# Up products by Strassen's algorithm on pairs of token chunks, with eight retention units ahead of the first product

## The reference

```python
state = gamma * state + einsum('bhd,bhe->bhde', k[:, :, t], v[:, :, t])
y[:, :, t] = scale * einsum('bhd,bhde->bhe', q[:, :, t], state)
# x = y, laid out as 3072 x 512
h = x @ w_in;  g = h * cos(h);  x = g @ w_out            # layer 1
h = x @ w_in                                             # layer 2
g = where(h >= 1, h, where(h <= -1, 0, (h + 1) ** 2 / 4))
out = g @ w_out
```

## Time and profile before

| what | value |
|---|---|
| median of 3 runs | 1165.73 us (1165.51 to 1165.99) |
| profiled execution, span | 1163.8 us |
| instructions in the profile | 14906 |
| PE, DVE, ACT, POOL busy | 1151.9, 556.8, 380.4, 132.4 us |
| mean granted TensorE clock | 0.997 of 2.4 GHz |
| DMA moved | 74.57 MB, 64 GB/s |

### The profile page before, as it was taken

One profiled execution on the slowest core, in us unless ns is written; L12 is line 12 of the kernel. 1 busy time (PEld: TensorE's weight loads), 2 busy tenths in 40 slices (PEclk: granted clock), 3 DMA queues, 4 the chain that ended last, 5 costly groups with the idle time before them and its releaser, 6 DMA issues.

```text
span 1163.8 us, 14906 instructions
## 1 busy us (share of the span) xinstructions
PE 1151.9 (99%) x5892; PEld 943.1 (81%) x5892; DVE 556.8 (48%) x836; ACT 380.4 (33%) x606; POOL 132.4 (11%) x113
## 2 busy tenths in 40 slices
PE   7999999999999999999999999999999999999998
PEld 5888888888888888788788888888888888888887
DVE  5555555556556555555554433433433433433433
ACT  2444332333333333323555322222222222222222
POOL 4445011001001010100354000000000000000000
PEclk8999999999999999999999999999999999999999
DMA  6433212022113112220452301001101001000100
GB/s 230 160 111 128 73 54 74 19 102 63 37 35 112 44 48 91 73 73 1 145 172 64 145 1 73 37 1 73 37 1 73 36 0 72 36 0 0 37 1 37
DMA packets 35481, 74.57 MB, mean 64 GB/s; under 512 B 3936, under 2 KB 4064, under 8 KB 33888
## 3 DMA queue, kind: packets, MB, share of 16 engines
q1 hardware_dynamic: 35424, 73.75, 18.7%
HBM read 54.86 MB, written 18.87 MB: 63 GB/s over the span
## 4 chain that ended last, share of the span: by engine, by line
PE 97%; DMA 1%; DVE 1%; SPq 0%; ACT 0%; issue 0%; DVEq 0%
PE up L378 45%; PE acc L401 23%; PE acc L403 22%; PE att L339 2%; PE att L318 2%; PE att L335 2%; PE att L359 1%; DMA raw<-in_w1u 0%; DMA q_sb<-in_q_t 0%; DVE x_lo L532 0%; PE acc L318 0%; PE att L354 0%; DVE am L471 0%; DVE x_lo L481 0%; DVE q_sb L461 0%
## 5 line engine op out<-in xcount | busy, mean ns | idle before, releaser
L378 PE MATMUL up<-x_hi,wu_hi 128*128 128x512 f32 x768 | 299.6, 390 | 1.1 <-DVE g_raw L514 1.1
L378 PE MATMUL up<-x_lo,wu_hi 128*128 128x512 f32 x768 | 298.8, 389 | 0.0
L378 PE MATMUL up<-x_hi,wu_lo 128*128 128x512 f32 x768 | 298.8, 389 | 0.0
L523 DVE SCALAR_TENSOR_TENSOR g_lo<-g_raw,g_hi 128x512 fp32r<-128x512 f32 x192 | 137.3, 715 | 181.9 <-ACT g_hi L608 181.9
L608 ACT ACTIVATE g_hi<-g_raw 128x512 fp32r<-128x512 f32 x192 | 121.3, 632 | 192.7 <-PE acc L403 108.8
L378 PEld LDWEIGHTS up<-x_hi,wu_hi 128*128 128x128 f32 x768 | 144.1, 188 | 32.8 <-DVE g_raw L514 2.5
L378 PEld LDWEIGHTS up<-x_hi,wu_lo 128*128 128x128 f32 x768 | 144.1, 188 | 30.0
L378 PEld LDWEIGHTS up<-x_lo,wu_hi 128*128 128x128 f32 x768 | 144.2, 188 | 29.7
L401 PE MATMUL acc<-g_hi,wd_hi 128*128 128x512 f32 x384 | 156.1, 406 | 0.0
L401 PE MATMUL acc<-g_hi,wd_lo 128*128 128x512 f32 x384 | 150.1, 391 | 0.0
L401 PE MATMUL acc<-g_lo,wd_hi 128*128 128x512 f32 x384 | 149.9, 390 | 0.0
(11 more groups left out here) (57 smaller groups left out, 899.5 us busy)
## 6 DMA issues: line engine op xcount, KB each, us to landing
q_sb<-in_q_t SPq DMA_DIRECT2D x24, 256.0 KB, 4.0
k_sb<-in_k_t SPq DMA_DIRECT2D x24, 256.0 KB, 4.0
x_hi_scratch<-x_hi SPq DMA_DIRECT2D x24, 256.0 KB, 3.0
x_lo_scratch<-x_lo SPq DMA_DIRECT2D x24, 256.0 KB, 3.4
x_hi<-x_hi_scratch SPq DMA_DIRECT2D x6, 1024.0 KB, 4.8
x_lo<-x_lo_scratch SPq DMA_DIRECT2D x6, 1024.0 KB, 6.9
kn<-in_k_n SPq DMA_DIRECT2D x22, 256.0 KB, 2.9
v_sb<-in_v_n SPq DMA_DIRECT2D x20, 256.0 KB, 2.6
```

Source lines behind the costliest of these rows:

```text
L378: last = nc.tensor.matmul(up[j % 2][:, :], w[:, j, k, :], x[:, par, k, :], start=(k == 0 and x is x_hi and w is wu_hi), stop=(k == KT - 1 ...
L523: nc.vector.scalar_tensor_tensor(out=g_lo[:, s, :], in0=g, scalar=2.0 if layer == 1 else 1.0, in1=g_hi[:, s, :].bitcast(F32), op0=ALU.mult ...
```

## The change

The unit of work becomes a *round*: two chunks of tokens in one layer (three rounds in layer 1, then three in layer 2, `s` in the code). The tokens of the two chunks, the two halves of the contraction and the two halves of the hidden features make a 2x2 by 2x2 block product, which is done by Strassen's algorithm in Winograd's form: 7 block products for 8. A *quad* (`q`, 8 in a round) is the four hidden tiles of feature tiles q and q+8 for both chunks. Its 7 products have 2 contraction tiles of three matmuls, 6 matmuls each. Some results are summed by PE in PSUM (p2 on p1, p7 and p4 on p6, p3 on p5), others by DVE. The hidden tiles other than the first are now in SBUF.

- POOL forms three sums of weight blocks for each contraction tile (`t_sums`, four operations of 128x128) and the low part of all seven (`t_low`, 128x896). ACT writes the high part (`t_high`). The up weights are no longer kept: they are loaded and split again for each quad of each round. The down weights are still kept (`wd_high`, `wd_low`, 128x1024 at a time, in round 0 one beside each quad).
- POOL forms sums of x blocks (8 operations of 128x512 a round), ACT and DVE split 14 tiles a round (`split_high`, `split_low`).
- ACT copies p1 out of PSUM and does the `turns`, which DVE did before. DVE gets `sum_u2`, `sum_u3`, `sum_h22`, `sum_h21`, `sum_h12`.
- Down products of the first chunk run beside the quads (two in a quad, from the second quad on). The rest, the whole second chunk's among them, follow the quads as a *tail* of 18 down products; `late` holds the second chunk's g until then.
- Retention: eight units (two chunks) run ahead of round 0's first product, from their own buffers; in rounds 0 and 1, eight more run in the tail. The last four units don't update the state. Layer 1's output goes to HBM as one float32 tensor, and is split again when read back.

The diff is long; its core, with new functions in the form they have after the change:

```diff
-        def walk(eng, body):            # one chunk after the other, 16 tiles each
+PRODUCTS = ["p1", "p6", "p2", "p7", "p5", "p4", "p3"]
+TAIL = [(1, QUADS - 1), (2, LATE[0]), (2, LATE[1]), (1, FT - 1)] + [(2, f) for f in LATE[2:]]
+BETWEEN = [1, 1, 1, 1, 1, 1, 2]
 # PE
+            def product(s, q, name):
+                if q == 0:
+                    pe.wait_ge(xlo_done, NS * s + max(m for m in range(NS) if SPLITS[m][0] == name) + 1)
+                if name == "p2":
+                    pe.wait_ge(p1_copied, n + 1)
+                if name == "p7":
+                    pe.wait_ge(u2_done, n + 1)
+                if name == "p4":
+                    pe.wait_ge(u3_done, n + 1)
+                if name == "p3":
+                    pe.wait_ge(h22_done, n + 1)
...
+            for u in range(AHEAD):
+                outputs(u)
+                outer(u)
+                if u + 2 < AHEAD:
+                    scores(u + 2)
...
+                for q in range(QUADS):
+                    product(s, q, "p1")
+                    product(s, q, "p6")
+                    if q:
+                        down(s, 1, q - 1)
+                    product(s, q, "p2")
+                    product(s, q, "p7")
+                    product(s, q, "p5")
+                    if q:
+                        down(s, 1, q - 1 + QUADS)
+                    product(s, q, "p4")
+                    product(s, q, "p3")
+                tail = list(TAIL)
+                if s < PAIRS - 1:
+                    for _ in range(5):
+                        down(s, *tail.pop(0))
+                    scores(u)
+                    down(s, *tail.pop(0))
+                    for i in range(AHEAD):
+                        outputs(u + i)
+                        outer(u + i)
+                        if i + 1 < AHEAD:
+                            scores(u + i + 1)
+                            for _ in range(BETWEEN[i]):
+                                down(s, *tail.pop(0))
 # DVE
+            def finish(s, q):
+                angle(s, q, 2)
+                if q == QUADS - 1:
+                    gate_low(s, *TAIL[1])
+                angle(s, q, 3)
+            def quad(s, q):
+                if q:
+                    finish(s, q - 1)
+                sum_u2(s, q)
+                if q:
+                    gate(s, q - 1, 2)
+                    gate(s, q - 1, 3)
+                    gate_low(s, 1, q - 1 + QUADS)
+                angle(s, q, 0)
+                sum_u3(s, q)
+                gate(s, q, 0)
+                sum_h22(s, q)
+                gate_low(s, 1, q)
+                angle(s, q, 1)
+                gate(s, q, 1)
+                sum_h21(s, q)
+                sum_h12(s, q)
 # ACT
+            def quad(s, q):
+                if q:
+                    finish_turns(s, q - 1)          # turns 2, turns 3
+                copy_p1(s, q)                       # q == 0 waits for all 14 splits
+                if q == 0 and s:
+                    rows_second(s - 1)
+                if q:
+                    curve(s, q - 1, 2)              # Sin, Square
+                    curve(s, q - 1, 3)
+                    gate_high(s, 1, q - 1 + QUADS)
+                if more:
+                    t_high(2 * (QUADS * s + q + 1))
+                turns(s, q, 0)
+                curve(s, q, 0)
+                if more:
+                    t_high(2 * (QUADS * s + q + 1) + 1)
+                gate_high(s, 1, q)
+                turns(s, q, 1)
+                if s == 0:
+                    wd_high(0, q)
+                curve(s, q, 1)
 # POOL, for the next quad
+                        t_sums(i)
+                        t_sums(i + 1)
+                        t_low(i)
+                        t_low(i + 1)
+                    if s == 0:
+                        wd_low(0, q)
```

More of the change, by code:

```diff
@@ L405, in down_product @@
                         last.then_inc(rows_ready, 1)
-                if (layer, place) != (2, "last") or j < FT - 1:
+                if not (s == SPANS - 1 and half == 2 and closes):
                     last.then_inc(down_done, 1)
-            def retention(blk, layer, place, j):
-                if layer == 1 and place != "last" and j < 3 * KT:
-                    if j % 3 == 0:
-                        scores(blk + 1, j // 3, att)
-                    elif j % 3 == 1:
-                        outputs(blk + 1, j // 3, True, v_sb)
-                    else:
-                        outer(blk + 1, j // 3, kn, v_sb)
@@ new lines, in _ @@
+            act.wait_ge(halves, 1)
+            nc.scalar.activation(probe[:, :], half_one[:, :], ACT.Sin)
+            for u in range(AHEAD):
+                copy_x(u)
+                if u < 4:
+                    split_high(0, u)
+                if u == 4:
+                    t_high(0)
+                    t_high(1)
+                if u == 5:
+                    split_high(0, 4)
+                if u == 6:
+                    split_high(0, 5)
+                    split_high(0, 6)
+            for m in range(7, NS):
+                split_high(0, m)
```

1151 lines of the change are left out of this document (690 added, 461 removed).

## The result

The changed kernel takes 1203.8 us (median of 4, 1200.3 to 1205.9); the kernel before took 1165.6 us beside it (4, 1164.7 to 1166.0). The ratio is 1.033 (1.031 to 1.035): slower by 38 us, where 1185 was forecast. The profiled execution of after took 1205.87 us with a span of 1204.1.

A forecast was written before the change was run, and what follows sets the result against it. The kernel was taken as a full PE stream. Prologue 57, matmuls 979.3, retention 66.2, ring 38.7, first quads 3, layer 1's tails 15, layer 2 4.5, retention's latency 14, end 5.5: 1183.2 us span, 1185 median; range 1138 to 1213.

The forecast's parts named there:

- the lock: DVE operations with two SBUF inputs and POOL operations don't run together; lengthens layer 1's quads, 38.7 us in all.
- ring: ACT and DVE passing a quad's tiles in fixed order: 14.56 us against PE's 14.96, 16.2 with POOL, 18.0 in round 0.
- the ring is hidden: Rival: POOL's long operations fall elsewhere than ahead of gate_low, so 14.56 us stays under 14.96; 1140 us, chance 0.22.
- first quad: First quads of layer 1's rounds: p4 and p3 wait for sums behind ACT, 1 us each, 3 in all.
- The dear rival: Rival: POOL's 128-column operations cost 1.25 us each, not 0.45, lengthening the quads of both layers; 1275 us, chance 0.06.
- 1.5 us for that: Prologue: charge for PE's clock being granted at 0.50 in stretches after idling, moving the last outputs from 46 to 47.5.
- Mask 7: Prologue: DVE's mask of the last of eight retention units, put at 44 us after seven more steps of the chain.
- upper bound of 63: Prologue: its charge, taken as 57 us, would be 63 if PE stayed at half clock all through.
- 1.5 at the layer's change: Between layers: load_wd stands behind the store and reload of x on SP, and wd_high holds gate_high; 1.5 us.
- The term 0.2267: Pace of a matmul on PE in us, read from the kernel before; 4320 matmuls make 979.3 us.
- the late ring: Tails of layer 1: down (2,0) waits behind a ring 4.5 us late, 6 in round 0; 15 us in all.
- retention's latency: Tails with retention: ACT's and DVE's 4.9 us a unit against PE's 4.4; 0.9 us for 16 units, 14 in all.

The follow-up runs named there:

- e1: The changed kernel without POOL's t_low, PE's third matmul of each group reading the high part again; 1166.9 us.
- e5: e3 with t_high earlier in ACT's order, t_low held until behind gate_low, and round 0's wd_low cut in two and placed later; 1156.8 us.
- e10: The same kernel as e3, timed; 1198.6 us, ratio 1.0287 to the kernel before.
- e11: The same kernel as e5, timed in 10 runs; 1159.2 us, ratio 0.9963 to the kernel before.
- e8: e7 with 44 useless matmuls of 128 columns on PE, behind each prologue unit and ahead of the first p1; 1137.7 us.
- e3: The changed kernel with three small tensors allocated behind the shared part, so that the up weights' tiles begin at byte 193664, not 196352; 1193.6 us.
- e4: The changed kernel with POOL's weight sums for quad 1 waiting for the last of the 14 low parts; 1207.9 us.
- e2: e1 with the low parts of the down weights (wd_low) left out too; 1150.1 us.
- e6: e5 with layer 2's wd_high and wd_low moved from round 2's tail to beside round 3's quads; 1144.0 us.
- e12: The same kernel as e8, timed in 5 runs; 1137.6 us, ratio 0.9774 to the kernel before.
- e7: e6 with six of the prologue's ten last low parts moved ahead of the last update of the state; 1148.7 us.

## Why the prediction was right, and where it was off

**The direction and its reason were right.** The size was not: 19 us slower were forecast and 38 measured. The step that decided was the lock: ring under PE's period by the rows, over it as soon as POOL's `t_low` stands ahead of gate_low. Predicted 16.2 us a quad in rounds 1 and 2, measured 15.80 (13.93 for the first interval); predicted 18.0 in round 0, measured 18.0 to 18.2 (16.83 for the first). e1 took POOL's operation away, and the ring was hidden; e5 kept it and moved it, and the ring was hidden too. The rival "the ring is hidden" was 44.7 us under the forecast; its condition (POOL's long operations elsewhere) is what e5 built, and by e10 and e11 it gave some 36. So that rival was priced somewhat dear, and rejected for the right reason: `t_low`'s start is tied to ACT's order. Its level of 1140 was too low by the same terms as the forecast's own: e11 is at 1159.

**Part of the agreement is luck.** The prediction charged each of seven intervals a round with the ring's excess over 14.96 us. But between the first two copies PE has only 42 matmuls, 9.5 us, and the ring takes nearly its full time: 13.93 us in rounds 1 and 2, 4.4 over, for 2.2 charged (ring and first quad together). The other six cost 0.84 each, for 1.24 charged. The two errors cancel: 9.4 us over in such a round, for 9.7. In round 0 they don't (26.4 for 22.3), and there a tail with 9.9 us over its matmuls, for 13, brings the stage within 0.8.

**"The dear rival" fell.** Operations of 128 columns take 0.45 us on POOL where DVE leaves it alone, as taken. Beside DVE's they take 0.78 to 0.90, and the group's mean over the run is 0.69. (By the rival's own terms the sum was 1277, not 1275.)

```profile
L914 POOL TENSOR_TENSOR raw<-raw 128x128 f32<-128x128 f32 x96 | 66.1, 688 | 151.9 <-DMA raw<-in_w2u 111.7
L924 POOL TENSOR_TENSOR tw<-raw,tw 128x896 fp32r<-128x896 f32 x96 | 204.7, 2141 | 165.6 <-ACT tw L725 165.6
```

`t_low` was estimated at 2.2 from a 512-column row, and took 2.14.

**Mis-sized: the prologue**, +11.3 us, half of the miss. The step that failed is "1.5 us for that": I had read in the earlier trace rows that the clock was granted at 0.50 and 0.83 in stretches after PE had stood idle, and charged 1.5 us once, for a prologue with twice as many units in which PE idles in every one. Mask 7 was to end at 44, so start at 42.6. It started at 51.2 in after and at 43.4 in e8, at full clock. The arithmetic of the chain was right, and the clock cost some 7.8 us of it. (e8 has six x_lo moved as well, but behind that mask.) The mask's own chain leaves 0.8 of its 8.6 us unexplained, and 2.7 more lie behind it: from the last mask's end to the copy 16.15 us, for 13.4. 2.2 of these are the clock again: from the mask's end to the first of the ten low parts there are 5.9 us, at a granted clock of 0.50, and 3.7 in e3 at 1.00. The ten low parts took 10.15, for 9.75 by the prediction's prices (10 x 0.6 and 3 x 1.25 of POOL's). Those prices were too high and a term was missing: without quad 1's weight sums beside them they took 8.71 (e4), so the weight sums, which I had left out, cost 1.4. In all the clock makes about 10 of the 11.3. The upper bound of 63, for PE at half clock all through, was too low as well: after passed it by nearly 6.

**Mis-sized: the layer's change**, +8.2 us in round 2. The step was "1.5 at the layer's change, where load_wd stands behind the store and reload of x on SP, and wd_high then holds gate_high". The place was right; the timeline shows ACT waiting 4.5 us there. But ACT's wait, with what hung on it, cost about 6 us and not 1.5 (e2), and the step left out that four `wd_low` in a row are the lock's worst case, which the same text had worked out for round 0: 3.7 more (e1 to e2). By e6 this place was worth 10.6 us.

**Mis-sized: the pace of the up matmuls**, +6 in layer 2. The term 0.2267 was read from operands at another place in SBUF; in after it was 0.2328. A quad has 42 of them, 42 x 0.0061 = 0.26 us, and 15.25 - 14.96 is 0.29. In layer 1 it is hidden under the ring, which is why e10 gave back 5 us and not 2016 x 0.0061 = 12.3. In e10 the stages of layer 2 take 496.7 us, for 496.6 by the prediction.

**Slightly dear: retention and tails**, -4.9 in round 1. From the last p1 copy to the next round's first there are 102.4 us against 95.6 of matmuls: 6.8 for what I put at 11.5 (4.5 for the late ring, 7 for retention's latency). That is 4.7 of the 4.9.

**What the change spent.** 288 matmuls less are 65.3 us. Net it lost 38, so 103 us were spent. What the runs gave back without touching the algorithm: 5.2 for the weights' place (e10), 39.4 from e10 to e11 (some 36 by POOL's order, the rest ahead of the first copy), and 21.6 for the down weights and the prologue together (e12). The rest, 37 us, is what these edits left. By e12's stages: 9 in the prologue (56.65 for 27.5, less the 20.0 of retention moved into it), 14 in the tails with retention (105.3 and 103.0 us in rounds 0 and 1, for 98.4 and 95.6 of matmuls), and 3 to 4 in the other rounds' edges (three of 65.0 to 65.1 for 63.9). Most of the rest, 11, lies in layer 1's quads: first to last copy took 102.5 to 103.8 in e5 (102.5 to 103.2 in e12), for 163.2 - 63.9 = 99.3 of matmuls. Round 3's took 3 more, and the end 4 less than the 5.5 us of before.

## What to carry to other kernels

Before fewer matmuls are bought with work on other engines, lay out the ring of the others from measured pitches, and mark in it each DVE operation that reads two SBUF tiles and each POOL operation; where POOL is first, DVE ended 0.55 us behind it here. If the ring then exceeds the period, move POOL's long operations beside DVE's PSUM readers before giving up the algorithm: here that alone made some 36 us, where e10 had been 34 us behind the kernel before. Where PE stands in a chain of latencies and idles, expect the lower clock in every link, not once.

## What was not expected of the hardware

- **The pace of a matmul depends on where its operands lie.** 128x128 by 128x512, fp32r: 0.2328 us with the weights from byte 196352, 0.2265 from 193664, both at clock 1.00. Moving the kernel before's weights by 256 bytes changed nothing; a move by 128 wasn't tried, and the cause is open.
- **Useless matmuls shortened a stage.** With 44 more, the mean granted clock over the first 60 us was 1.00 in place of 0.90, and the first p1 copy came 4.7 us sooner (e7 to e8).
- **The port is passed to and fro.** Where both engines have work queued, they alternate by whole instructions: six low parts of 0.69 us took 7.27 (e7), ten took 10.15 to 10.53. POOL pays too: 0.45 us becomes 0.90, and `wd_low` 2.85 where it was 2.4 alone. The Trainium skill, "SBUF — State Buffer", section "SBUF: two separate sides", names the exclusive hold of the port; the traces here agree, and show that it costs both sides.
- An operation of DVE that reads and writes SBUF with one input (layer 2's clamp) takes 0.41 us for 512 columns; the ones that read PSUM take 0.69.
